# A fused retention, MLP and gated-attention kernel on one core: load buffers moved by 384 bytes, the first v on another queue, and a new order of the first projections and values

## What is computed

```python
# 1. retention: decayed linear attention, per head
state = gamma * state + outer(k[t], v[t]);  y[t] = scale * q[t] @ state
# 2. layer norm and MLP, 512 -> 2048 -> 512
x = x + relu(norm(x) * g_ln @ w_ch1) @ w_ch2
# 3. four experts of causal softmax attention (head size 64); a token takes the two
#    experts with the largest gate logits, weighted by the softmax of the two
logits = x @ w_gate
ye = softmax(causal(scale * (x @ wq[e]) @ (x @ wk[e]).T)) @ (x @ wv[e]) @ wo[e]
out = sum over the two chosen e of weight[e] * ye
```

## Time and profile before

| | us |
|---|---|
| median of 3 runs (lowest, highest) | 467.53 (466.18, 469.15) |
| the profiled execution | 467.75 |
| its span, first to last instruction | 466.0 |
| PE busy | 453.9 |
| DVE busy | 265.5 |
| POOL busy | 152.4 |
| ACT busy | 149.6 |

### The profile page before, as it was taken

One profiled execution on the slowest core, in us unless ns is written; L12 is line 12 of the kernel. 1 busy time (PEld: TensorE's weight loads), 2 busy tenths in 40 slices (PEclk: granted clock), 3 DMA queues, 4 the chain that ended last, 5 costly groups with the idle time before them and its releaser, 6 DMA issues.

```text
span 466.0 us, 7417 instructions
## 1 busy us (share of the span) xinstructions
PE 453.9 (97%) x2762; PEld 393.5 (84%) x2762; DVE 265.5 (57%) x588; ACT 149.6 (32%) x342; POOL 152.4 (33%) x188
## 2 busy tenths in 40 slices
PE   8899999999999999999999999999997999999997
PEld 7689988888888888888888888888997999998885
DVE  4655761285416388732275784144437688888854
ACT  2333541111112111111131111142436577777753
POOL 1165639999700000000003000001802266665650
PEclk9999999999999999999999999999999899999999
DMA  7999514444100000000042000000144443344114
GB/s 160 218 210 198 150 46 134 134 127 130 41 1 1 0 0 0 0 0 0 0 112 48 0 1 0 0 2 0 24 103 114 102 99 96 94 108 97 53 47 181
DMA packets 65791, 32.99 MB, mean 71 GB/s; under 512 B 47584, under 2 KB 61920, under 8 KB 65760
## 3 DMA queue, kind: packets, MB, share of 16 engines
q1 hardware_dynamic: 64960, 32.38, 28.6%
q10 hardware_dynamic: 800, 0.20, 0.2%
HBM read 19.98 MB, written 3.15 MB: 50 GB/s over the span
## 4 chain that ended last, share of the span: by engine, by line
PE 89%; DMA 3%; SPq 2%; issue 2%; DVE 2%; ACT 1%; POOL 1%; ACTq 0%; POOLq 0%
PE ps L742 28%; PE ps L751 28%; PE ps L827 7%; PE ps L880 4%; PE ps L846 4%; PE ps L798 4%; PE ps L861 4%; PE ps L904 3%; DMA raw_q<-in_q 3%; PE ps L650 2%; PE ps L637 2%; PE ps L657 2%; PE ps L627 1%; SPq L464 1%; SPq L427 1%
## 5 line engine op out<-in xcount | busy, mean ns | idle before, releaser
L1309 DVE SCALAR_TENSOR_TENSOR h_t_lo<-ps,h_t_hi 128x512 fp32r<-128x512 f32 x48 | 33.2, 692 | 125.1 <-ACT h_t_hi L1030 125.1
L1030 ACT ACTIVATE h_t_hi<-ps 128x512 fp32r<-128x512 f32 x48 | 28.7, 598 | 215.7 <-PE ps L742 215.7
L742 PE MATMUL ps<-xn_t_hi,w_hi 128*128 128x512 f32 x192 | 74.8, 390 | 0.0
L742 PE MATMUL ps<-xn_t_lo,w_hi 128*128 128x512 f32 x192 | 74.8, 390 | 0.0
L742 PE MATMUL ps<-xn_t_hi,w_lo 128*128 128x512 f32 x192 | 74.7, 389 | 0.0
L751 PE MATMUL ps<-w_hi,h_t_hi 128*128 128x512 f32 x192 | 74.7, 389 | 0.0
L751 PE MATMUL ps<-w_lo,h_t_hi 128*128 128x512 f32 x192 | 74.7, 389 | 0.0
L751 PE MATMUL ps<-w_hi,h_t_lo 128*128 128x512 f32 x192 | 74.7, 389 | 0.0
L590 POOL TENSOR_SCALAR a<-a,inv_den,weight 128x768 f32<-128x768 f32 (+5 forms) x48 | 34.2, 722 | 56.2 <-DVE inv_den L1478 30.3
L742 PEld LDWEIGHTS ps<-xn_t_lo,w_hi 128*128 128x128 f32 x192 | 36.1, 188 | 8.0 <-DVE xn_t_lo L1269 0.6
L751 PEld LDWEIGHTS ps<-w_hi,h_t_hi 128*128 128x128 f32 x192 | 36.1, 188 | 7.5
(11 more groups left out here) (149 smaller groups left out, 881.4 us busy)
## 6 DMA issues: line engine op xcount, KB each, us to landing
raw_w<-in_moe_w_ch SPq DMA_DIRECT2D x32, 256.0 KB, 2.9
k_twice_hi<-pj_hi SPq DMA_DIRECT2D x32, 96.0 KB, 2.2
k_twice_lo<-pj_lo SPq DMA_DIRECT2D x32, 96.0 KB, 2.2
out_y<-out_sb SPq DMA_DIRECT2D x12, 256.0 KB, 2.1
raw_k<-in_k SPq DMA_DIRECT2D x7, 384.0 KB, 6.1
raw_q<-in_q SPq DMA_DIRECT2D x7, 384.0 KB, 6.2
raw_v<-in_v SPq DMA_DIRECT2D x7, 384.0 KB, 6.0
q_both<-pj_hi SPq DMA_DIRECT2D x16, 96.0 KB, 2.1
```

What stands on the lines that cost most here:

```text
L742: mm = pe.matmul(ps[:, f % 2, :], w1[a_][:, f, kk, :], xn_t[b_][:, kk, :], start=(kk == 0 and p_ == 0), stop=(kk == KT - 1 and p_ == 2))
L1030: act.activation(h_t["hi"][:, f % 2, :], ps[:, f % 2, :], ACT.Relu).then_inc(s_hhi, 1)
L1309: dve.scalar_tensor_tensor(h_t["lo"][:, f % 2, :], ps[:, f % 2, :], 0.0, f32(h_t["hi"][:, f % 2, :]), ALU.max, ALU.subtract).then_inc(s_hl ...
```

## The change

Six edits.

1. A dummy tensor of 384 bytes a partition is put behind the decay table. All buffers behind it start 384 bytes later; `raw["q"]`, `raw["k"]` and `raw["v"]` now start at multiples of 512.
2. SP's start: k first, then the small decay table, then the rest; the four v pieces leave SP. ACT issues v of pair 0 as two DMAs of 192 KB after it has waited for the first q.
3. POOL scales all of pair 1 and pair 2; DVE scales pair 0 alone.
4. PE turns pair 1 ahead of both `state_outputs` of pair 0; ACT's `y_out(0, .)` moves behind its copies of pair 1.
5. Values go by batch entry, all six of the first and then all six of the second; two `turn_last` each follow `values(0)` and `values(1)`; projections 0 to 3 and scores 0 to 2 are put among the values; `row_max(2)`, `exponent(2, .)` and `sums(2)` come before cycle 0; the gate is worked in two halves, the second around `project(4)`.
6. In the cycles with fewer than two pieces, ACT and DVE do `a_t_hi`/`a_t_lo` of the second turn before the single projection (cycle 5), before `output_out` (cycles 6, 7) and before `exponent(3c+3, 0)` (cycle 6).

```diff
+        sb(ctx, "raw_at_512", [P, 2 * HP * 2 * NC])
@@ SP
-            sp.dma_start(decay[:, :, 0:1, :], tables[:, :, 0:1, :]).then_inc(s_tab, 16)
             for n, g in FIRST:
...
+                if (n, g) == FIRST[0]:
+                    sp.dma_start(decay[:, :, 0:1, :], tables[:, :, 0:1, :]).then_inc(s_tab, 16)
@@ ACT
+            act.wait_ge(s_first["q"][0], 32)
+            for j in range(2):
+                act.dma_start(raw["v"][:, 0, j], heads["v"][0][:, j]).then_inc(s_first_v, 16)
@@ POOL
-            for n in range(2, NIT):
+            pool.wait_ge(s_tab_rest, 16)
+            for n in range(1, NIT):
                 scale_pair(n)
@@ PE, stage 1
             for g in range(2):
                 chunk_outputs(0, g)
-                state_outputs(0, g)
             for unit in range(4):
                 turn(1, unit)
+            for g in range(2):
+                state_outputs(0, g)
@@ PE, stage 3
-        V_TILES = [(b, c) for b in range(B) for c in range(DONE)]
-        V_TILES += [(b, c) for b in range(B) for c in range(DONE, NC)]
-        EARLY = B * DONE
+        V_TILES = [(b, c) for b in range(B) for c in range(NC)]
+        EARLY = NC + 1
...
+            values(0); turn_last(0); turn_last(1); values(1); turn_last(2); turn_last(3)
+            values(2); project(0); values(3); project(1); values(4); values(5)
+            project(2); values(6); project(3); scores(0); values(7); values(8)
+            scores(1); values(9); scores(2); values(10); values(11); project(4)
@@ DVE, stage 3 (one call a line in the code)
+            ...; values_lo(5); gate_in(0); gate_rank(0); project_lo(2); gate_out(0)
+            values_lo(6); project_lo(3); row_max(0); values_lo(7); sums(0); values_lo(8)
+            row_max(1); values_lo(9); row_max(2); sums(1); values_lo(10); sums(2)
+            values_lo(11); gate_in(1); gate_rank(1); project_lo(4); gate_out(1)
@@ ACT, cycle(c)
-                if g + 3 < LAST:
+                if c <= HALVES - 3:
                     exponent(g + 3, 0)
-                if len(fill) > 0:
+                if len(fill) > 1:
                     project_hi(fill[0])
                 for w in range(2):
                     a_t_hi(g + 1, w)
+                if len(fill) == 1:
+                    project_hi(fill[0])
+                if c == HALVES - 2:
+                    exponent(g + 3, 0)
```

More of the change, by code:

```diff
@@ L530, in scale_pair @@
                 for g in range(2):
[L531 to L535, removed]
+                    for which in "kq":
+                        if n == 1 and g == 0:
+                            pool.wait_ge(s_scaled[which], 2)
                         if n >= RB and g == 0:
@@ L941, in cycle @@
                     scores(g + 5)
[L943 to L946, removed]
-            project(0, range(KT))
+            values(0)
+            turn_last(0)
+            turn_last(1)
+            values(1)
+            turn_last(2)
+            turn_last(3)
+            values(2)
+            project(0, range(KT))
+            values(3)
+            project(1, range(KT))
+            values(4)
+            values(5)
+            project(2, range(KT))
             values(6)
[L949 to L952, removed]
+            project(3, range(KT))
             scores(0)
-            project(3, range(KT))
+            values(7)
+            values(8)
             scores(1)
+            values(9)
             scores(2)
+            values(10)
+            values(11)
             project(4, range(KT))
@@ L1145, in _, with gate_exp @@
             act.activation(w_o["hi"][:, :, :], raw_wo[:, :, :], ACT.Copy).then_inc(s_wohi, 1)
[L1146 to L1152, removed]
-            project_hi(0)
-            values_hi(6)
[L1156 to L1160, removed]
+            def gate_exp(b):
+                units = slice(b * NC, (b + 1) * NC)
+                act.wait_ge(s_gin, b + 1)
+                act.activation(weight[:, units, :], shifted[:, units, :], ACT.Exp).then_inc(s_gexp, 1)
+            values_hi(0)
+            last_hi(0)
+            last_hi(1)
+            values_hi(1)
+            last_hi(2)
+            last_hi(3)
+            values_hi(2)
+            project_hi(0)
+            values_hi(3)
+            project_hi(1)
+            values_hi(4)
+            values_hi(5)
+            gate_exp(0)
+            project_hi(2)
+            values_hi(6)
+            project_hi(3)
             exponent(0, 0)
+            values_hi(7)
             exponent(0, 1)
-            project_hi(3)
+            values_hi(8)
             exponent(1, 0)
+            values_hi(9)
             exponent(1, 1)
+            exponent(2, 0)
+            values_hi(10)
+            exponent(2, 1)
+            values_hi(11)
+            gate_exp(1)
             project_hi(4)
@@ L1435, in gate_out @@
-            def gate_out():
-                dve.wait_ge(s_gexp, 1)
-                gate.then(dve.tensor_tensor(weight[:, :, :], weight[:, :, :], rank[:, :, :], ALU.mult))
-                gate.then(dve.tensor_reduce(top[:, :, 0], weight[:, :, :], AX.X, ALU.add))
-                gate.then(dve.tensor_scalar(top[:, :, :], top[:, :, :], SOFTMAX_EPS, None, ALU.add))
-                gate.then(dve.reciprocal(top[:, :, :], top[:, :, :]))
-                dve.tensor_tensor(weight[:, :, :], weight[:, :, :],
-                                  top[:, :, :].broadcast_to((P, B * NC, E)), ALU.mult).then_inc(s_weight, 1)
+                    gate.counted(dve.tensor_tensor(beats[:, units, j + 1:E, j],
+                                                   logits[:, units, j:j + 1].broadcast_to(each(n)),
+                                                   logits[:, units, j + 1:E], ALU.is_ge))
@@ L1522, in cycle @@
                     project_lo(fill[1])
-            for t in range(6):
-                values_lo(t)
-                if 1 <= t <= KT:
-                    last_lo(t - 1)
-            project_lo(0)
-            values_lo(6)
-            project_lo(1)
-            for t in range(7, B * NC):
-                values_lo(t)
-            gate_in()
-            gate_rank()
-            project_lo(2)
-            gate_out()
+            values_lo(0)
+            last_lo(0)
+            last_lo(1)
+            values_lo(1)
+            last_lo(2)
+            last_lo(3)
+            values_lo(2)
+            project_lo(0)
+            values_lo(3)
+            project_lo(1)
+            values_lo(4)
+            values_lo(5)
+            gate_in(0)
+            gate_rank(0)
+            project_lo(2)
+            gate_out(0)
+            values_lo(6)
+            project_lo(3)
             row_max(0)
+            values_lo(7)
             sums(0)
-            project_lo(3)
+            values_lo(8)
             row_max(1)
+            values_lo(9)
+            row_max(2)
             sums(1)
+            values_lo(10)
+            sums(2)
+            values_lo(11)
+            gate_in(1)
+            gate_rank(1)
             project_lo(4)
+            gate_out(1)
             for c in range(HALVES):
```

77 lines of the change are left out of this document (42 added, 35 removed).

## The result

| | before | after |
|---|---|---|
| median, us (lowest, highest; executions) | 468.31 (466.18, 469.15; 4) | 461.78 (461.71, 461.87; 4) |
| span of the profiled execution | 466.0 | 459.8 |
| PE busy in it | 453.9 | 451.2 |

The account below looks back on a forecast made before the run. PE was taken to bound the kernel, busy 453.9 of 466.0 us. Gains of 2.0 + 3.4 + 1.0 = 6.4 us took the median from 467.53 to a forecast 461.1 us, range 457.9 to 464.6.

Parts of the forecast that it names:

- Term 1: Start of stage 1: faster loads of q, k and v remove PE's idle time from 15.6 to 28.5 us, worth 2.0 us.
- `key_values(0)` later than 9.5 us: Stage 1, first pair: a start this late, from v arriving late, would show the forecast wrong.
- 270 GB/s or more from 12 to 17 us: Stage 1 loads: the DMA rate that would show the faster loads had come, against 221 GB/s before.
- The rule that was weighed there: Stage 1 loads: rows not starting at multiples of 256 bytes pay an extra transaction; aligned rows would reach 301 GB/s.
- rival A: Stage 1: the loads don't get faster, leaving 4.8 us of gain in all, 462.7 us; chance 0.27.
- Term 2: Head of stage 3: PE's 2.66 us hole and the slow matmuls behind it go, less a new wait; 3.4 us.
- a sign against it: Stages 1 and 3: ACT's two DMA issues over 0.7 us each, or PE waiting for evictions among the values.
- Term 3: Last cycles of stage 3: the waits of 0.28 and 0.74 us before turn_a in cycles 5 and 6 go, 1.0 us.
- B: Head of stage 3: the hole only moves and the clock falls again, gain 3.0 us, 464.5 us; chance 0.11.
- C: Stage 1: the clock falls to 1.2 GHz at the start and stays there, slower, up to 483 us; chance 0.04.
- D: Whole kernel, better: no wait in cycle 0 and pair 0 sooner, gain 8.2 us, 459.3 us; chance 0.12.

## Why the prediction was right

**The sum.** 6.4 us were forecast and 461.1 us; the profiled spans give 6.2 and the median is 461.78. The sum held only what happens in the span; the 0.35 us more outside it make up half of the 0.7 us by which the median is missed. By its terms: 2.0 forecast and 1.94 found up to the MLP, 3.4 and 3.57 up to the first `attend`, 1.0 and 0.73 after it. The causes are the ones that were named; that the sum came so close has some luck in it, as errors of 0.3 to 0.4 us inside the terms offset each other.

**Term 1, right in size, with a share in the wrong place.** The loads became faster as leaned to, 279 to 290 GB/s in the steady slices with edit 1 alone and 300 by the issue times, nearer the upper bound of 295 than the 221 of before, and PE's idle time in the window fell by 2.25 us. Booked for edit 2 were 0.4 us, and 0 for the stretch to 15.6 us with an end of -0.7. Found was a loss of 0.60 us there, by the route that the text named: v shares the engines with pair 1, `key_values(0)` goes at 9.37 us instead of 8.84 and `chunk_outputs(0,1)` waits for the mask. The step that failed is the crediting of edit 2's freed DMA time as a gain while its later v was booked at nothing. The two belong together, and the run without edits 2 to 4 shows that they cancel. The late v can cost more: the sign "`key_values(0)` later than 9.5 us" stayed away in the changed kernel (9.37, 9.23 and 9.22 us in three executions), but with the same order of loads it started at 10.83 without edit 6, where stage 1 lost 1.46 us. The sign "270 GB/s or more from 12 to 17 us" failed too, with 261, 265 and 256 in three executions of the changed kernel, and said nothing on the time: the mean holds slices of 235 and 249, from which PE no longer had to wait.

The rule that was weighed there (the Trainium skill, DMA: Bandwidth & Descriptors, How a descriptor splits into AXI transactions) was right in that rows that don't start on a multiple of 256 cost more, and its estimate of 301 GB/s is near the 300 GB/s of the issue times and above the 279 to 290 of the slices. If its beats held for the writing side, a row 32 bytes off would need 9 of them instead of the 12 of one 128 bytes off, with the three cycles a packet of the same page (Why small descriptors are slow) 12 instead of 15, so an estimate of 276 GB/s from the 221 measured at 128 bytes off. The run with rows 32 bytes off has 221 from 12 to 17 us, too. The measurement decides: here a cut row costs the same at both places of the cut.

The 285 GB/s of misplaced rows, which spoke for rival A, were read as a rate that lasts. The slices around it say otherwise: the two before it, 46 to 48 us, have 33 and 166 GB/s. In all four traces with cut rows, until 49 us, a slice of 1 us over 250 GB/s (253 to 299) stands only within 2 us behind one under 190; in the steady stretch from 12 to 17 us the slices have 211 to 234. With edit 1 alone 279 to 290 last for 7 us. The larger packets of that slice, a tenth of their number, were also about a fifth of its bytes. Why the first 2 us after a lull are faster isn't shown.

**Term 2, right.** The hole and the low clock are gone, PE waits 0.2 us before `project(0)` (0.3 forecast) and in cycle 0. That wait was forecast at 0.8 to 1.0 and the chain that causes it was the right one; moving the gate shows it to be worth 0.61 us, of which the row shows 0.37 as a wait. What the text named as a sign against it stayed away: ACT's two DMA issues take 0.50 us each, and among the values nothing holds PE but those 0.2 us. The forecast took the cost of the low clock from one execution and put it at 1.80 us; by the same matmuls at full clock it is 1.55, because the six scores behind a hole take 1.12 us and not the 0.87 of a later cycle that they were compared with. Booked were 4.46 - 1.0; found are 2.6 for the hole and 1.5 for the clock, less 0.6, 3.5 us: two mis-sized prices that cancel. By the table above the low clock of that execution is also what the typical one pays, 465.8 - 464.3 = 1.5 us of span, and that was luck: a median of before in another group would have moved the result by 1.5 us either way.

**Term 3, mis-sized.** 1.0 us forecast, 0.7 measured by the cycles. Both waits of the earlier trace rows went, but `a_t_lo` of the third turn, behind which DVE is now late, holds `attend` for 0.30 and 0.26 us. The step that failed was to take the removed waits as the gain without walking on to the next reader of the same engine.

**The rivals.** A and B are refuted by the runs above. C did not happen: the granted clock is 1.00 in all windows of stage 1, though PE had waits of 0.83 and 0.97 us there. D was too hopeful by the pair-0 loss, the wait in cycle 0 and term 3.

## What to carry to other kernels

Start the buffer that a DMA fills with rows of 256 bytes on a multiple of 512 bytes of the partition before touching the order of the loads: one dummy tensor was worth 1.9 us, edits 2 to 4 nothing beside it. When a wait is taken away, follow the same engine to its next reader and book what is left after that; and when a hole in PE's work stands beside a low clock, read the spans of several executions by their mean clock before giving the hole a price.

## What the runs showed of the hardware

- 256-byte rows cut by a 256-byte boundary load at 221 GB/s from 12 to 17 us, whether 32 or 128 bytes lie behind the cut; the same rows in buffers that start on a multiple of 512 at 283 with edit 1 alone (279 to 290 in steady slices). An issue of 384 KB then takes 1.31 instead of 1.75 us.
- The same rows in buffers that start 256 bytes behind a multiple of 512 have the same 1.31 us an issue but more and longer stretched issues between, and lose about 0.8 us of the whole time by the medians of eight and sixteen executions.
- Cut rows reach 253 to 299 GB/s only in slices of 1 us within 2 us behind a slice under 190; in the steady slices from 12 to 17 us they have 211 to 234.
- In every variant one to three issues of SP in the start's stream take 2.1 to 3.2 us (2.97 at 14.36 us before, 2.95 at 7.08 and 2.20 at 15.86 after). Behind the one that begins between 14 and 17 us mostly, not always, stands a slice in which the engines deliver 65 to 161 GB/s (146 before, 141 after, 201 without edit 1). Nothing in the trace shows why.
- One and the same hole of PE, 2.63 and 2.66 us long, left the granted clock at 1.00 in one profiled execution and at 0.72 in the other, where the matmuls behind it took 1.55 us more. The unchanged kernel has a third group of executions, about 3 us above the first, at mean clocks of 0.991 and 0.993; that the hole is the cause there isn't shown.
